# Linear attention and two MLPs: the steps of the second network's weight split set to 1, 4, 7 and 11 of each chunk, its store first in SP's turn, one last store moved to ScalarE's queue

## Chip, cores and metric

The kernel is one program on 1 core of a Trainium2 chip. The metric is the device time of one execution in microseconds (us), the lower the better. Runs of one kernel lie within about 0.2% of each other.

## What is computed

All tensors are float32. Cut to what matters (B = 8 batches, H = 8 heads, S = 576 positions, 64 values per head; 4608 tokens of 512 values; a first network 512 to 2048 to 512, a second 512 to 1024 to 512):

```python
q_s = softmax(q, axis=-1)          # over the 64 values of a head
k_s = softmax(k, axis=2)           # over the 576 positions
kv = einsum('bhsd,bhse->bhde', k_s, v)
x = einsum('bhsd,bhde->bhse', q_s, kv)      # then heads beside each other: 4608 x 512
h = x @ w_in
g = maximum(h, 0) + alpha * minimum(h, 0)
x2 = g @ w_out
h = x2 @ w_in2
sm = softmax(h, axis=-1)
solu = h * sm
ln = (solu - mean(solu)) / sqrt(var(solu) + 1e-6) * g_ln
out = ln @ w_out2
```

## The kernel before, in words

Every large product is made of three matmuls of 128 x 128 by 128 x 512 in float32r: an operand is split into a high half (ScalarE copies it, rounded) and a low half (VectorE or POOL subtracts the high half from the value), and high x high, high x low and low x high are added in PSUM.

The first network's upper product runs in 9 chunks c of 512 tokens, 16 steps f each (`up(c, f)`, lines 1965 to 1967, twelve matmuls). Chunks 0 to 7 hold the first 512 positions of batches 0 to 7, the last one all remainders. A step's result lies in one of four PSUM banks of `ps_y`. ScalarE makes the negative part into `gst` (`negative`, line 993), VectorE adds the rest (`prelu`, line 1421 in the program, called "the negative's sum" below), and SP stores `gst` to `g_scratch` (`store_g`, line 478). `gst` has three buffers: the negative of step f waits until the store of step f - 3 has landed. `up` of step f waits for the sum of step f - 4.

Between the steps of chunks 0 to 6 the attention of the next batch, b = c + 1, is worked on, each engine in an order written out by hand, `for f in range(NF)` with `if f == ...`:

- SP loads K in step 3 (`load_k`), stores qz, the blockwise transposed q, in steps 7 and 8 (`store_qz`, line 500), loads Q of the batch after in step 8 (`load_q`, lines 414 and 419), and loads q back, transposed, as QN in 16 transfers of 64 KB, five each in steps 9 to 11 and the last in step 12 (`load_qz`, line 508). V comes in steps 12 to 15. All of it goes through SP's one queue, in program order; a wait of SP holds whatever follows.
- VectorE makes the q sums in steps 3 and 4 (lines 1387 to 1393), subtracts the maxima of K in step 5 (lines 1345, 1349), transposes q in pairs of blocks in steps 6 and 7 (line 1401), norms kv in step 10 (line 1364), makes kvl in step 11.
- ScalarE makes the exponentials of K in step 7 (`k_exp`, line 940), the two halves of kvh in step 11 (lines 952, 953), copies qR in step 12 (line 959), makes the high halves qTh of q in steps 12 and 13 (`q_high`, line 969).
- POOL makes their low halves qTl (line 812).
- TensorE makes the kv product after step 9 (line 1901), needs the first two of the three K exponentials for it, transposes q's remainder after step 11 (line 1914), multiplies it after step 13 (`xr_product`, line 1950, which needs qR), and makes the attention product in four parts after steps 14 and 15 (`x_product`, lines 1939 to 1941).

Besides, chunks 1 to 6 split the second network's weights, 22 pieces in all, at four steps of each chunk, here called the split. For a piece n, ScalarE makes the high half into `whl` (`ws_high`, lines 1002 and 1004) once the store of piece n - 1 has landed, since `whl` is one buffer; VectorE makes the low half (`ws_low`, lines 1427 and 1430) and for some pieces turns a buffer of weights into a difference (`ws_turn`, lines 1441 and 1450); SP stores both halves, 512 KB, to `ws_scratch` (`store_ws`, line 473) one step later. The raw weights come into `wst` in four loads of 1 MB (`load_ws`, lines 464 and 468), each after the last piece that reads what it overwrites:

```python
WS_AT = (1, 6, 10, 13)
WS_LOADS = {(0, 15): 0, (2, 11): 1, (4, 7): 2, (5, 7): 3}
```

A key (c, f) of the second table is SP's turn in which the load is issued. The pieces 7, 14 and 18 are the first that read the loads 1, 2 and 3. SP's turn of a step ends so:

```python
if f == 15:
    store_xr(b)
if (c, f) in WS_LOADS:
    load_ws(WS_LOADS[c, f])
if ws_piece(c, f - 1) is not None:
    store_ws(ws_piece(c, f - 1))
```

After the chunks come the first network's lower product and the second network, which the change doesn't touch but for the last line: `store_out` (line 687) stores the remainders' output rows, two stores of 64 rows per tile, all from SP. The last tile is made by `out_copy(17, 1)` (line 1191) on ScalarE.

Of the kernel before, what the change touches and what calls it, by code (L numbers as in the profile page):

```python
# [26 lines left out]
def linear_attention_two_mlps(nc, q, k, v, w_in, w_out, alpha, w_in2, w_out2, g_ln, out):  # L27
# [29 lines left out]
    with ExitStack() as ctx:  # L57
# [244 lines left out]
        SUM_AT = {1: 0, 2: 1, 3: 2, 6: 3}  # L302


        WS_AT = (1, 6, 10, 13)
        WS_W2, WS = 14, 14 + NF2
        WS_LOADS = {(0, 15): 0, (2, 11): 1, (4, 7): 2, (5, 7): 3}
        WS_SUMS = (1, 1, 2, 3, 3, 4, 4)

        class Piece:  # L310
# [101 lines left out]
        def _(sp):  # L412
# [119 lines left out]
            for c in range(B - 1):  # L532
                b = c + 1
                for f in range(NF):
                    if c == 0 and f + 4 < NF:
                        load_w(f + 4)
                    if f > 0:
                        store_g(c, f - 1)
                    if c == 0 and 3 <= f <= 7:
# [29 lines left out]
                        store_xr(b)  # L569
                    if (c, f) in WS_LOADS:  # L570
                        load_ws(WS_LOADS[c, f])
                    if ws_piece(c, f - 1) is not None:
                        store_ws(ws_piece(c, f - 1))
                store_g(c, NF - 1)
                if b + 1 < B:
                    load_v_part(b + 1, TT)
# [104 lines left out]
            def store_out(n, t):  # L681
                u, r = pair_at(n)
                sp.wait_ge(o_ok, 2 * n + t + 1)
                if u == PAIRS:
                    for i in range(2):
                        b = 2 * (2 * t + r) + i
                        sp.dma_start(out[b * S + TOK:(b + 1) * S, :], ost[i * REM:(i + 1) * REM, t, :]).then_inc(o_st[t], 16)
                else:
                    rows_out = out.rearrange("(b s) n -> b s n", b=B)[2 * u + t, 0:TOK, :]
                    sp.dma_start(rows_out.rearrange("(p t) n -> p t n", t=TT)[:, r, :], ost[:, t, :]).then_inc(o_st[t], 16)  # L690
# [243 lines left out]
        def _(act):  # L934
# [104 lines left out]
            for c in range(B - 1):  # L1039
                b = c + 1  # L1040
                for f in range(NF):
                    if c == 0 and f + 3 < NF:
                        w_high(f + 3)
                    negative(c, f)
                    if f == (3 if c == 0 else 2):
                        q_exp(b, 0)
                        q_exp(b, 1)
                    if f == (4 if c == 0 else 3):
                        q_exp(b, 2)
                    if f == 7:  # L1050
                        for piece in range(3):
                            k_exp(b, piece)
                    if ws_piece(c, f) is not None:
                        ws_high(ws_piece(c, f))
                    if f == 11:
                        kv_high(b)
                    if f == 12:
                        qr_copy(b)
                    if f == (13 if c == 0 else 12):
                        q_high(b, 0)  # L1060
                        q_high(b, 1)
                    if f == (14 if c == 0 else 13):
                        q_high(b, 2)
                        q_high(b, 3)
                    if f == 14:
                        xr_copy(b)
                        x_high(b, 0)
                        x_high(b, 1)
                    if f == 15:
                        x_high(b, 2)  # L1070
                        x_high(b, 3)
# [216 lines left out]
            out_copy(16, 1)  # L1288
            out_copy(17, 0)
            out_copy(17, 1)  # L1290


        @block.vector
        def _(dve):
# [204 lines left out]
            for c in range(B - 1):  # L1499
                b = c + 1  # L1500
                for f in range(NF):
# [38 lines left out]
                        kv_norm(b)  # L1540
                    if f == 11:
                        kv_low(b)
                    if ws_piece(c, f) is not None:
                        ws_low(ws_piece(c, f))
                        ws_turn(ws_piece(c, f))
                    if c == 0 and f == 13:
                        q_low_second(0)
                        q_low_second(1)
                    if b + 1 < B:
# [4 lines left out]
                            k_rem(b + 1)  # L1554
                        if f == 11:
                            k_blocks(b + 1)
                    if f == 14:
                        x_low(b, 0)
                        x_low(b, 1)
# [586 lines left out]
```

## Time and profile before

| | |
|---|---|
| median of 3 runs | 1207.49 us (1205.42 to 1207.53) |
| the profiled execution's own time | 1208.86 us |
| its span | 1207.1 us |
| TensorE busy | 1187.6 us, 98% |
| VectorE, ScalarE, POOL busy | 74%, 45%, 26% |
| SP's hardware queue | 212.5 MB, 56.4% of 16 engines' span |

Times in the trace count from the span's start. The profiled execution is a fourth one, and the 1.8 us by which its own time exceeds the span lie around the program. PE is TensorE's matmuls, DVE VectorE, ACT ScalarE, SPq the issuing of SP. A matmul's own time of 0.39 us overlaps its neighbours: one starts every 0.227 us at the full clock. "[1.64 <-POOL ...]" is the time that an engine stood idle before an instruction, and what ended it. "To landing" is the time from a DMA's issue to its completion count.

### The profile page before, as it was taken

To read this page: it belongs to the slowest core of one execution; us is meant where nothing else is said; L and a number is where in the kernel's file an instruction comes from. 1 tells how busy PE (TensorE), PEld (TensorE's weight loads), DVE (VectorE), ACT (ScalarE), POOL (GpSimd) and SP (SyncE) were. 2 spreads that over 40 slices of the span, in tenths; PEclk is the share of its full clock that TensorE was granted. 3 is DMA by queue.
4 is the path that set the end of the run, shared out by engine and by line. 5 is a ranking of instruction groups with operands and counts; after the bars stand their busy time and mean duration, and the time that the engine had idled before them with its cause. 6 is when DMAs were issued, how large, how long until landed. Compare 5 with 4: busy or idle time off the path is not lost.

```text
span 1207.1 us, 16162 instructions
## 1 busy us (share of the span) xinstructions
PE 1187.6 (98%) x6013; PEld 982.4 (81%) x6013; DVE 891.2 (74%) x1165; ACT 538.2 (45%) x744; POOL 309.1 (26%) x233
## 2 busy tenths in 40 slices
PE   7999999999999999999999999999999999999998
PEld 6878887887888888888888888898788888888886
DVE  7768777786775475977769777686898787878772
ACT  4534534434354344443444344443556464545452
POOL 5722414132242000000000000036544535353310
PEclk8999999999999999999999999999999999999999
DMA  9998877869874735264270542498346545454444
GB/s 231 255 259 260 244 254 217 271 202 273 270 237 166 266 133 191 96 205 144 83 239 28 189 159 70 142 290 266 122 149 192 176 134 174 136 177 130 145 153 129
DMA packets 211918, 225.07 MB, mean 186 GB/s; under 512 B 63208, under 2 KB 148224, under 8 KB 211712
## 3 DMA queue, kind: packets, MB, share of 16 engines
q1 hardware_dynamic: 206064, 212.50, 56.4%
q0 software_dynamic: 5728, 11.53, 3.3%
q8 instruction: 47, 0.77, 0.3%
q14 instruction: 31, 0.25, 0.1%
q10 hardware_dynamic: 48, 0.01, 0.0%
HBM read 128.51 MB, written 95.48 MB: 186 GB/s over the span
## 4 chain that ended last, share of the span: by engine, by line
PE 83%; DVE 8%; DMA 4%; issue 2%; SPq 2%; ACT 1%; POOL 0%; ACTq 0%; DVEq 0%
PE ps_y L1965 9%; PE ps_y L1966 9%; PE ps_y L1967 9%; PE ps_y L2051 5%; PE ps_y L2053 5%; PE ps_y L2055 5%; PE ps_y L2109 5%; PE ps_y L2111 5%; PE ps_y L2110 5%; PE ps_m L2053 3%; PE ps_m L2055 3%; PE ps_m L2051 3%; PE ps_m L2090 2%; PE ps_m L2094 2%; PE ps_m L2092 2%
## 5 line engine op out<-in xcount | busy, mean ns | idle before, releaser
L1965 PE MATMUL ps_y<-X,W 128*128 128x512 f32 x576 | 227.2, 394 | 0.0
L1967 PE MATMUL ps_y<-X,W 128*128 128x512 f32 x576 | 224.6, 390 | 0.0
L1966 PE MATMUL ps_y<-X,W 128*128 128x512 f32 x576 | 224.6, 390 | 0.0
L1421 DVE SCALAR_TENSOR_TENSOR gst<-gst,nslope,ps_y 128x512 f32<-128x512 f32 x144 | 104.4, 732 | 113.4 <-ACT gst L993 113.0
L993 ACT ACTIVATE gst<-ps_y 128x512 f32<-128x512 f32 x144 | 85.8, 596 | 225.6 <-PE ps_y L1967 166.4
L854 POOL TENSOR_TENSOR x2r<-x2r 128x256 f32<-128x256 f32 x18 | 25.2, 1401 | 406.9 <-DMA x2r<-x_scratch 406.9
L1965 PEld LDWEIGHTS ps_y<-X,W 128*128 128x128 f32 x576 | 108.4, 188 | 23.5
L1967 PEld LDWEIGHTS ps_y<-X,W 128*128 128x128 f32 x576 | 108.3, 188 | 22.9
L1966 PEld LDWEIGHTS ps_y<-X,W 128*128 128x128 f32 x576 | 108.4, 188 | 21.8
L2051 PE MATMUL ps_y<-rh,WOc 128*128 128x512 f32 (+1 forms) x320 | 117.9, 369 | 1.1 <-DVE rl L1583 1.1
L2053 PE MATMUL ps_y<-rl,WOc 128*128 128x512 f32 (+1 forms) x320 | 117.7, 368 | 0.0
L2055 PE MATMUL ps_y<-rh,WOc 128*128 128x512 f32 (+1 forms) x320 | 117.7, 368 | 0.0
L2109 PE MATMUL ps_y<-WO,zh 128*128 128x512 f32 x288 | 112.3, 390 | 1.7 <-DVE zl L1727 1.7
L2111 PE MATMUL ps_y<-WO,zl 128*128 128x512 f32 x288 | 112.1, 389 | 0.0
L2110 PE MATMUL ps_y<-WO,zh 128*128 128x512 f32 x288 | 112.1, 389 | 0.0
L1095 ACT ACTIVATE rh<-RX 128x1024 fp32r<-128x1024 f32 x54 | 57.4, 1062 | 85.8 <-PE ps_y L2055 41.7
L1095 ACT ACTIVATE rh<-RY 128x1024 fp32r<-128x1024 f32 x54 | 57.4, 1062 | 81.6 <-PE ps_y L2055 55.7
L1583 DVE TENSOR_TENSOR rl<-RX,rh 128x1024 fp32r<-128x1024 f32 x54 | 66.2, 1225 | 34.2 <-ACT rh L1095 34.2
L1583 DVE TENSOR_TENSOR rl<-RY,rh 128x1024 fp32r<-128x1024 f32 x54 | 67.4, 1250 | 28.0 <-ACT rh L1095 27.9
L882 POOL TENSOR_TENSOR x2lb<-x2r,x2hb 128x1792 fp32r<-128x1792 f32 x18 | 75.1, 4171 | 41.9 <-ACT x2hb L1130 41.9
L1185 ACT ACTIVATE zh<-zt 128x1024 fp32r<-128x1024 f32 x36 | 38.0, 1056 | 88.4 <-PE ps_y L2111 58.9
L812 POOL TENSOR_TENSOR qTl<-QN,qTh 128x512 fp32r<-128x512 f32 x26 | 33.2, 1298 | 155.3 <-ACT qTh L969 155.3
(189 smaller groups left out, 2534.6 us busy)
## 6 DMA issues: line engine op xcount, KB each, us to landing
g_scratch<-gst SPq DMA_DIRECT2D x144, 256.0 KB, 3.6
RX<-g_scratch SPq DMA_DIRECT2D x36, 512.0 KB, 3.6
z_scratch<-zb SPq DMA_DIRECT2D x36, 512.0 KB, 3.5
zt<-z_scratch SPq DMA_DIRECT2D x144, 128.0 KB, 2.8
ws_scratch<-whl SPq DMA_DIRECT2D x22, 512.0 KB, 4.5
RY<-g_scratch SPq DMA_DIRECT2D x18, 512.0 KB, 4.6
RZ<-g_scratch SPq DMA_DIRECT2D x18, 512.0 KB, 4.7
x2r<-x_scratch SPq DMA_DIRECT2D x18, 512.0 KB, 5.1
```

Source lines behind the costliest of these rows:

```text
L1095: nc.scalar.activation(t.tile(rh), t.raw(src), ACT.Copy).then_inc(bh_ok, 1)
L1421: nc.vector.scalar_tensor_tensor(gst[:, n % 3, :], gst[:, n % 3, :], nslope[:, f:f + 1], ps_y[:, f % 4, :], ALU.mult, ALU.add).then_inc(g_ ...
L1583: nc.vector.tensor_tensor(t.tile(rl), t.raw(src), t.tile(rh).bitcast(F32), ALU.subtract).then_inc(bl_ok, 1)
L1965: nc.tensor.matmul(o, W1[:, f, 0, a, :], x[:, 0, a, :], start=(a == 0), stop=False)
L1966: nc.tensor.matmul(o, W1[:, f, 0, a, :], x[:, 1, a, :], start=False, stop=False)
L1967: mm = nc.tensor.matmul(o, W1[:, f, 1, a, :], x[:, 0, a, :], start=False, stop=(a == KT - 1))
L2051: nc.tensor.matmul(o, WOc[k][:, 0, kt, cols], hi[:, s, :], start=begin, stop=False, skip_group_check=more)
L2053: nc.tensor.matmul(o, WOc[k][:, 0, kt, cols], lo[:, s, :], start=False, stop=False, skip_group_check=more)
L2055: mm = nc.tensor.matmul(o, WOc[k][:, 1, kt, cols], hi[:, s, :], start=False, stop=end, skip_group_check=more)
L2109: nc.tensor.matmul(o, zh[:, t, f * P:(f + 1) * P], WO2[:, f, 0, :], start=(f == 0), stop=False)
L2110: nc.tensor.matmul(o, zh[:, t, f * P:(f + 1) * P], WO2[:, f, 1, :], start=False, stop=False)
L2111: mm = nc.tensor.matmul(o, zl[:, t, f * P:(f + 1) * P], WO2[:, f, 0, :], start=False, stop=(f == NF2 - 1))
```

## The change

The split's four steps move from 1, 6, 10, 13 to 1, 4, 7, 11. The loads 1, 2 and 3 move with the pieces that they wait for: from step 11 of chunk 2 to step 8, from step 7 of chunks 4 and 5 to step 5. SP takes the split's store as the first thing of its turn instead of the last. In ScalarE's step 7 the split's high half now stands ahead of the three K exponentials, and in step 11 behind kvh. VectorE takes the low half behind the K maxima and blocks of its step. At the end one of the four stores of the last two tiles' rows goes out from ScalarE behind its last copy.

```diff
--- before.py
+++ after.py
@@ -302,9 +302,9 @@
         SUM_AT = {1: 0, 2: 1, 3: 2, 6: 3}
 
 
-        WS_AT = (1, 6, 10, 13)
+        WS_AT = (1, 4, 7, 11)
         WS_W2, WS = 14, 14 + NF2
-        WS_LOADS = {(0, 15): 0, (2, 11): 1, (4, 7): 2, (5, 7): 3}
+        WS_LOADS = {(0, 15): 0, (2, 8): 1, (4, 5): 2, (5, 5): 3}
         WS_SUMS = (1, 1, 2, 3, 3, 4, 4)
 
         class Piece:
@@ -534,6 +534,8 @@
                 for f in range(NF):
                     if c == 0 and f + 4 < NF:
                         load_w(f + 4)
+                    if ws_piece(c, f - 1) is not None:
+                        store_ws(ws_piece(c, f - 1))
                     if f > 0:
                         store_g(c, f - 1)
                     if c == 0 and 3 <= f <= 7:
@@ -569,8 +571,6 @@
                         store_xr(b)
                     if (c, f) in WS_LOADS:
                         load_ws(WS_LOADS[c, f])
-                    if ws_piece(c, f - 1) is not None:
-                        store_ws(ws_piece(c, f - 1))
                 store_g(c, NF - 1)
                 if b + 1 < B:
                     load_v_part(b + 1, TT)
@@ -682,7 +682,7 @@
                 u, r = pair_at(n)
                 sp.wait_ge(o_ok, 2 * n + t + 1)
                 if u == PAIRS:
-                    for i in range(2):
+                    for i in range(1 if 2 * n + t == TILES - 1 else 2):
                         b = 2 * (2 * t + r) + i
                         sp.dma_start(out[b * S + TOK:(b + 1) * S, :], ost[i * REM:(i + 1) * REM, t, :]).then_inc(o_st[t], 16)
                 else:
@@ -1047,13 +1047,13 @@
                         q_exp(b, 1)
                     if f == (4 if c == 0 else 3):
                         q_exp(b, 2)
+                    if f == 11:
+                        kv_high(b)
+                    if ws_piece(c, f) is not None:
+                        ws_high(ws_piece(c, f))
                     if f == 7:
                         for piece in range(3):
                             k_exp(b, piece)
-                    if ws_piece(c, f) is not None:
-                        ws_high(ws_piece(c, f))
-                    if f == 11:
-                        kv_high(b)
                     if f == 12:
                         qr_copy(b)
                     if f == (13 if c == 0 else 12):
@@ -1288,6 +1288,8 @@
             out_copy(16, 1)
             out_copy(17, 0)
             out_copy(17, 1)
+            act.wait_ge(o_ok, TILES)
+            act.dma_start(out[B * S - REM:B * S, :], ost[REM:P, 1, :]).then_inc(o_st[1], 16)
 
 
         @block.vector
@@ -1540,9 +1542,6 @@
                         kv_norm(b)
                     if f == 11:
                         kv_low(b)
-                    if ws_piece(c, f) is not None:
-                        ws_low(ws_piece(c, f))
-                        ws_turn(ws_piece(c, f))
                     if c == 0 and f == 13:
                         q_low_second(0)
                         q_low_second(1)
@@ -1554,6 +1553,9 @@
                             k_rem(b + 1)
                         if f == 11:
                             k_blocks(b + 1)
+                    if ws_piece(c, f) is not None:
+                        ws_low(ws_piece(c, f))
+                        ws_turn(ws_piece(c, f))
                     if f == 14:
                         x_low(b, 0)
                         x_low(b, 1)
```

SP's queue in chunk 2, steps 7 to 9, before (ws_scratch is the split's store, g_scratch a step's result, wst the raw weights):

```order
L500 DMA qz_scratch<-qz 128x1024
L473 DMA ws_scratch<-whl 128x2x512
L478 DMA g_scratch<-gst 128x512
L500 DMA qz_scratch<-qz 128x1024
L414 DMA Q<-q_dram 64x8x64
L419 DMA Q<-q_dram 128x4x256 x2
L478 DMA g_scratch<-gst 128x512
L508 DMA QN<-qz_scratch 32x4x128 x5
```

The same now:

```order
L500 DMA qz_scratch<-qz 128x1024
L473 DMA ws_scratch<-whl 128x2x512
L478 DMA g_scratch<-gst 128x512
L500 DMA qz_scratch<-qz 128x1024
L414 DMA Q<-q_dram 64x8x64
L419 DMA Q<-q_dram 128x4x256 x2
L464 DMA wst<-w_in_dram 128x1024 x2
L478 DMA g_scratch<-gst 128x512
L508 DMA QN<-qz_scratch 32x4x128 x5
```

The store stands at the same place but is that of the piece of step 7, no more of step 6; and the two 512 KB loads stand behind Q and ahead of the g store of step 8.

SP's queue in chunk 2, steps 11 and 12, before:

```order
L478 DMA g_scratch<-gst 128x512
L508 DMA QN<-qz_scratch 32x4x128 x5
L464 DMA wst<-w_in_dram 128x1024 x2
L473 DMA ws_scratch<-whl 128x2x512
L478 DMA g_scratch<-gst 128x512
L508 DMA QN<-qz_scratch 32x4x128
```

The same now:

```order
L478 DMA g_scratch<-gst 128x512
L508 DMA QN<-qz_scratch 32x4x128 x5
L473 DMA ws_scratch<-whl 128x2x512
L478 DMA g_scratch<-gst 128x512
L508 DMA QN<-qz_scratch 32x4x128
```

The loads are gone from here; the store ahead of the last QN transfer is that of the piece of step 11 instead of step 10.

ScalarE in chunk 4, steps 4 to 11, before (gst are the negatives, whl the split's high half, KK the K exponentials, kvh the two halves of kv):

```order
L993 ACTIVATE gst<-ps_y 128x512 x3
L1002 ACTIVATE whl<-wst 128x512
L993 ACTIVATE gst<-ps_y 128x512
L940 ACTIVATE KK<-KK 64x512
L940 ACTIVATE KK<-KK 128x1024 x2
L993 ACTIVATE gst<-ps_y 128x512 x3
L1004 ACTIVATE whl<-wst,acols 128x512
L993 ACTIVATE gst<-ps_y 128x512
L952 ACTIVATE kvh<-kvf 64x4x64
L953 ACTIVATE kvh<-kvf 64x4x64
```

The same now:

```order
L993 ACTIVATE gst<-ps_y 128x512
L1002 ACTIVATE whl<-wst 128x512
L993 ACTIVATE gst<-ps_y 128x512 x3
L1004 ACTIVATE whl<-wst,acols 128x512
L940 ACTIVATE KK<-KK 64x512
L940 ACTIVATE KK<-KK 128x1024 x2
L993 ACTIVATE gst<-ps_y 128x512 x4
L952 ACTIVATE kvh<-kvf 64x4x64
L953 ACTIVATE kvh<-kvf 64x4x64
L1004 ACTIVATE whl<-wst,acols 128x512
```

The first piece that reads load 2 has moved from step 10 to step 7, ahead of the K exponentials, and a further one stands behind kvh in step 11.

## Rows read from the trace of the kernel before

**Rows 1.** Windows, chunks 1, 2, 4, 5: length, busy, PEclk, DMA share, GB/s
```profile
85.14:136.59 51.45, 51.45 (x305) 41.89 (x304) 40.25 (x58) 21.98 (x38) 14.94 (x10) 1.00 0.87 266
136.59:192.09 55.50, 53.57 (x305) 42.87 (x304) 38.60 (x57) 21.87 (x38) 15.16 (x10) 0.97 0.79 244
...
243.55:295.87 52.32, 51.55 (x305) 41.89 (x304) 39.73 (x56) 22.04 (x39) 15.19 (x10) 1.00 0.82 249
295.87:347.57 51.70, 51.54 (x305) 41.89 (x304) 37.58 (x55) 22.35 (x38) 15.19 (x10) 1.00 0.83 257
```

**Rows 2.** Timeline of TensorE, chunks 2 and 4: start, us, operation, idle
```profile
176.22 0.68 PE L1950 MATMUL ps_m<-qR,kvf 64*64 64x64 f32 x16
...
185.57 0.50 PE L1939 MATMUL ps_m<-qTh,kvh 128*128 128x512 f32 x1 [1.64 <-POOL qTl L812]
...
188.27 0.63 PE L1965 MATMUL ps_y<-X,W 128*128 128x512 f32 x1
...
267.92 3.58 PE L1901 MATMUL ps_m<-V,KK 128*64 128x65 f32 x80
...
277.95 0.46 PE L1914 MATMUL ps_m<-ident,QN 64*128 64x64 f32 x4 [0.78 <-DVE kvf L1364]
```

**Rows 3.** Timeline of ScalarE, chunk 2, steps 11 to 13
```profile
170.25 0.60 ACT L993 ACTIVATE gst<-ps_y 128x512 f32<-128x512 f32 x1 [1.60 <-PE ps_y L1967]
170.75 0.40 ACT L952 ACTIVATE kvh<-kvf 64x256 fp32r<-64x256 f32 x1
...
174.10 0.38 ACT L959 ACTIVATE qR<-ps_m 128x256 f32<-128x256 f32 x1
...
181.37 0.63 ACT L1002 ACTIVATE whl<-wst 128x512 fp32r<-128x512 f32 x1 [4.44 <-DMA ws_scratch<-whl]
183.54 1.15 ACT L969 ACTIVATE qTh<-QN 128x512 fp32r<-128x512 f32 x2 [1.55 <-DMA QN<-qz_scratch]
```

**Rows 4.** Chain that ended last, chunks 2 and 4: start, us, what
```profile
175.59 7.93 DMA QN<-qz_scratch
...
266.58 9.10 DMA g_scratch<-gst
```

**Rows 5.** Timeline of SP's queue, chunk 2
```profile
158.31 0.37 SPq L473 DMA_DIRECT2D ws_scratch<-whl  x1
...
173.66 0.91 SPq L464 DMA_DIRECT2D wst<-w_in_dram  x2
```

**Rows 6.** Windows within chunk 2, columns as in rows 1
```profile
161.00:170.00 9.00, 9.00 (x105) 7.36 (x104) 4.68 (x8) 1.72 (x3) 0.00 (x0) 1.00 0.98 302
170.00:176.00 6.00, 6.00 (x29) 4.75 (x28) 5.80 (x9) 3.34 (x7) 0.78 (x1) 1.00 0.79 219
```

**Rows 7.** Timeline of VectorE, chunks 2 and 4
```profile
157.64 0.64 DVE L1427 TENSOR_TENSOR whl<-wst,whl 128x512 fp32r<-128x512 f32 x1
...
159.47 1.28 DVE L1401 STREAM_TRANSPOSE qz<-QN 128x512 f32<-128x512 f32 x2
...
258.00 0.65 DVE L1421 SCALAR_TENSOR_TENSOR gst<-gst,nslope,ps_y 128x512 f32<-128x512 f32 x1
```

**Rows 8.** DMA issues, 163 to 164 and 265 to 265.7: us to landing
```profile
g_scratch<-gst SPq DMA_DIRECT2D x1, 256.0 KB, 6.4
...
wst<-w_out_dram SPq DMA_DIRECT2D x1, 1024.0 KB, 6.8
```

**Rows 9.** DMAs issued in 1202 to 1208
```profile
out_dram<-ost SPq DMA_DIRECT2D x4, 128.0 KB, 2.4
```

**Rows 10.** Timeline of ScalarE, chunks 4 and 5
```profile
261.85 0.60 ACT L993 ACTIVATE gst<-ps_y 128x512 f32<-128x512 f32 x1 [4.10 <-DMA g_scratch<-gst]
...
263.34 2.52 ACT L940 ACTIVATE KK<-KK 64x512 f32<-64x512 f32 x3
...
312.90 0.60 ACT L993 ACTIVATE gst<-ps_y 128x512 f32<-128x512 f32 x1 [2.83 <-DMA g_scratch<-gst]
```

**Rows 11.** Timeline of SP's queue at the end
```profile
1202.48 2.38 SPq L687 DMA_DIRECT2D out_dram<-ost  x4
```

## The prediction

> **What bounds the kernel now.** I began with the windows by chunk, because the change touches only the first network's chunks 1 to 6 and the very end. A chunk that nothing disturbs takes 51.45 us and TensorE is busy in all of it [rows 1]: there the matmuls set the time, and no work saved on another engine is worth anything. Chunk 2 takes 55.50, chunk 4 52.32 and chunk 5 51.70. Above 51.45 that is 4.05, 0.87 and 0.25, together 5.17 us. This is all that a better order of steps could give back there; chunks 1, 3 and 6 can only lose.
>
> Next, where the 5.17 us arise. In chunk 2 TensorE stands 1.64 us before the product of step 15, which waits for qTl, and soon after, single matmuls take 0.63 us where 0.39 was usual: the granted clock fell to half [rows 2]. Behind the wait stands ScalarE: the high half of the weight split of step 13 idles 4.44 us for the split's last store, then qTh idles 1.55 us for a transfer of QN, and only then can POOL make qTl [rows 3]. That transfer, the sixteenth of its kind, was issued at 175.59 and took 7.93 us to land [rows 4], since SP had put two 512 KB loads at 173.66 ahead of it [rows 5]. In chunk 4 it is a g store that took 9.10 us behind the 1 MB load: the negative of step 10 waited for it, and through it the kv norm and the transpose at 277.95, before which TensorE stood 0.78 us [rows 2, 4]. Chunk 5 repeats it, milder. So SP's queue and the 16 DMA engines are the true second resource: they are busy 0.98 of the time from 161 to 170 [rows 6].
>
> **Part 1, what goes away.** No split stands between the negative of step 13 and qTh of chunk 2 any more, and the load leaves step 11: the 1.64 us wait and the half clock lose their cause, 4.05 us. The 1 MB loads of chunks 4 and 5 leave step 7, so that the g store that step 10 needs isn't behind them: 0.87 and 0.25 us. No bytes are removed and no instruction is cheaper; all is moved.
>
> **Part 2, the new waits in chunk 2.** SP issues in order, so a store that comes first in its turn holds everything behind it until VectorE has made its low half. In step 8 this store now belongs to the piece of step 7, whose low half comes after the second pair of transposes. The pair ends at 159.47 + 1.28 = 160.75 as before (the piece's low half and the turn behind it moved from ahead of it to step 4), the low half 0.64 later [rows 7], so the store goes out at about 161.4 and not 158.31 [rows 5]: 3.1 us later, and with it the g store of step 7, qz, the Q loads and the g store of step 8. Before, the latter was issued in the stretch 163 to 164 and took 6.4 us [rows 8], so it landed at 170.1. The engines were at 0.98 [rows 6], so a shift is hardly absorbed; I take 2.1 of the 3.1 (some slack lay ahead of 159). Then the new load lies before it: a 1 MB load took 6.8 us to land [rows 8], of which some 2 us are the way of any transfer here (the last stores of the kernel, 128 KB each, took 2.4 [rows 9]), so it occupies 2.4 to 4.4; I take 3.4. The g store of step 8 lands at 170.1 + 2.1 + 3.4 = 175.6. The negative of step 11 needs its buffer: 175.6 and not 170.25 [rows 3]. Behind it on ScalarE come two halves of kvh (the first 0.40), now also the split's high half (0.63), the negative of step 12 (0.60) and the copy to qR (0.38 [rows 3]); as each starts some 0.1 before the last one ends, 2.8 us. TensorE wants qR at 176.22 [rows 2], so the point is a landing at 173.4, and at 175.6 it stands 2.2 us (bounds 0, if the load is absorbed, and 3.9). Behind it the last QN transfer follows the store of the piece of step 11, which waits for a low half that is itself late: about 0.5 us at the product of step 15 (0 to 1). Whether the clock halves after a wait of 2.2 us is open: it did after 1.64 us and didn't after the 0.78 us of chunk 4 [rows 2]. At eight matmuls by about 0.2 us it is 1.6, and I count half, 0.8. Chunk 2: 2.2 + 0.5 + 0.8 = 3.5 us in place of 4.05.
>
> **Part 3, the new waits in chunks 4 and 5.** The load at step 5 can only follow the low half of step 4's piece: VectorE reaches the negative's sum of step 5 at 258.00 [rows 7], the low half now goes in ahead of it, so the store is issued at 258.7, the g store of step 4 behind it, the load at 259.5. The queue is then behind the K loads: the g store of step 3 landed at 261.85 [rows 10]. After it store and g store need about 2 us, the load 2.4 to 4.4: it lands at 266.3 to 268.3, mean 267.3. ScalarE now makes the high half of that piece in step 7 ahead of the three K exponentials (2.52 us [rows 10]), where before it made them from 263.34 with no wait. TensorE's kv product starts at 267.92 [rows 2] and needs the first two, 2.1 us after the load with the split's 0.6. So 267.3 + 2.1 = 269.4, a stand of 1.4 us (0 to 2.4). In chunk 5 the g store of step 3 landed 17.0 us into the chunk against 18.3 in chunk 4 [rows 1, 10], 1.3 earlier, and the kv product starts at the same place: 0.2 us (0 to 1.1). Chunk 1 has the same shift of step 8 without a load: 0.1 us (0 to 0.5).
>
> Here a rule speaks otherwise. The row has 6.8 us for 1 MB behind a half full queue. The Trainium skill, DMA: Bandwidth & Descriptors, section Anatomy of one DMA, gives a fixed 2.0 us plus the bytes at 436 GB/s, an estimate of 4.4 us for 1 MB, while its section Bandwidth lists 6.15 us measured; the trace agrees with the second. By the first, both the loads' new places would be harmless in chunks 4 and 5.
>
> **Part 4, the last rows.** SP issues four stores of 128 KB one after the other from 1202.48, 2.38 us in all, each landing 2.4 us later [rows 9, 11]. One of them now goes from ScalarE, whose last copy they wait for. The last landing moves up by one issue, 2.38 / 4 = 0.6 us (0 if both queues share the issuing hardware, which no row shows).
>
> **Sum.** Before 5.17. After: 3.5 + 1.4 + 0.2 + 0.1 = 5.2. The chunks stay as they are, the end gives 0.6. The sum is made against the profiled execution, 1208.86 us (span 1207.1 and 1.8 around it), 1.37 above the median of 1207.49: 1208.3 on its scale, 1206.9 on the median's. About 0.2%, 2.4 us, is what can be told from no change: faster means below 1205.1, slower above 1209.9.
>
> **The rivals.**
> 1. The queue drains. The load at step 8 and the later stores find gaps, since the bytes are spread better than in a row at 173.66. At 2.4 us for the load and no delay of the negative of step 11, all chunks run at 51.45: 5.17 + 0.6 less, 1201.7; with a rest of 1.2 + 0.5 us in chunk 2 it is 1203.4. For it: from 170 to 176, with the qz loads being issued, the engines were at 0.79 [rows 6]. Against: 0.98 in just the stretch that the load enters [rows 6]. Chance 0.30.
> 2. The queue doesn't drain, and the kernel is slower. One mechanism: the negative of step 11 of chunk 2 waits for the g store behind Q and the load. It decides at 173.4; at 177.3 TensorE stands 3.9 us, the clock halves (1.6) and 0.5 follows, 6.0 in place of 4.05; with the loads' upper bound the K exponentials cost 2.4 and 1.1 too and chunk 1 0.1. Then 9.6 - 5.17 - 0.6 = +3.8: 1211.3. For it: in chunk 4 a g store with a load and a split's store just ahead took 9.10 us [rows 4]. Chance 0.20.
> 3. The change doesn't do what it says: the split's bytes still lie ahead of the last QN transfer, which lands no earlier than 183.5, and only the 0.6 us of the end are left: 1206.9. Chance 0.05, within the no-change band.
>
> **How the numbers follow.** The forecast, waits that move from one place to another, has 0.45, with a range of its own of 1204.5 to 1209.5. Faster is rival 1 and a small part of the forecast, 0.33. Slower is rival 2 and a small part, 0.22. The rest is 0.45. The range leaves out the lowest tenth (chunks wholly clean on a lucky chip) and the highest: 1202.0 to 1210.5. I name 1206.9.
>
> **What would show it.** In the windows by chunk, chunk 2 at about 55, chunk 4 near 52.8, chunk 5 near 51.7, chunk 1 within 0.3 of 51.45. In chunk 2 no idle of qTh behind the split; instead an idle of several us before the negative of step 11 with a g store as its releaser, and a TensorE gap before the product into qR's buffer. In chunks 4 and 5 the high half of step 7 ends an idle behind the 1 MB load, and the kv product starts over 1 us late in chunk 4. At the end three stores from SP and one from ScalarE. The prediction is wrong if the negative of step 11 starts before 173.4 in chunk 2's own time (36.8 us into it), or if the half clock appears in chunk 4.

## The result, and the profile after

| | before | after |
|---|---|---|
| median (range, runs) | 1207.34 us (1205.42 to 1207.53, 4) | 1221.11 us (1216.93 to 1222.97, 4) |
| the profiled execution, its span | 1208.86, 1207.1 us | 1216.93, 1215.1 us |

The change makes the kernel slower, by a ratio of 1.0113 with an interval of 1.0084 to 1.0142: some 14 us where I had forecast none. The profiled execution of the changed kernel is the fastest of its four and that of the kernel before lies 1.5 us above its median, so the traces show only 8.0 us of it. The windows of the changed kernel, chunks 1 to 6 in order, with the columns of [rows 1]:

```profile
84.84:138.30 53.46, 52.09 (x305) 41.74 (x304) 40.59 (x58) 21.41 (x39) 15.46 (x10) 1.00 0.84 254
138.30:195.46 57.16, 54.18 (x305) 43.93 (x304) 40.76 (x57) 21.75 (x38) 15.91 (x10) 0.94 0.77 239
195.46:247.44 51.98, 51.85 (x305) 41.84 (x304) 38.95 (x57) 21.70 (x38) 15.51 (x10) 1.00 0.78 237
247.44:300.50 53.06, 51.62 (x305) 41.81 (x304) 40.23 (x56) 22.07 (x38) 15.94 (x10) 1.00 0.81 251
300.50:355.71 55.21, 51.97 (x305) 41.73 (x304) 38.12 (x55) 21.99 (x38) 15.97 (x10) 1.00 0.80 245
355.71:407.16 51.45, 51.45 (x305) 41.88 (x304) 30.35 (x48) 21.24 (x36) 15.51 (x10) 1.00 0.48 160
```

Nearly all of it is in these chunks. Against [rows 1], chunk 1 is 2.01 us longer, chunk 2 1.66, chunk 4 0.74 and chunk 5 3.51; chunk 3, which ran at 51.46 before, is 0.52 longer. That is 8.4; chunk 1 starts 0.30 earlier than before and all that follows chunk 6 is 0.13 shorter, its gain of 0.5 at the very end included, so the spans differ by 8.0. TensorE's busy time exceeds 51.45 by 2.73 us in chunk 2 and by at most 0.64 in the others, where most of the loss is standing. Where it waits, in the timeline of TensorE, twice in chunk 1, then in chunks 2, 4 and 5:

```profile
110.01 2.20 PE L1903 MATMUL ps_m<-V,KK 128*64 128x65 f32 x47 [0.73 <-ACT KK L940]
...
133.32 0.50 PE L1941 MATMUL ps_m<-qTh,kvh 128*128 128x512 f32 x1 [0.35 <-POOL qTl L812]
...
180.97 1.12 PE L1952 MATMUL ps_m<-qR,kvf 64*64 64x64 f32 x16 [2.98 <-issue]
182.02 0.79 PE L1967 MATMUL ps_y<-X,W 128*128 128x512 f32 x1
182.62 0.63 PE L1968 MATMUL ps_y<-X,W 128*128 128x512 f32 x1
...
273.32 1.83 PE L1903 MATMUL ps_m<-V,KK 128*64 128x65 f32 x40 [1.44 <-ACT KK L940]
...
327.91 3.58 PE L1903 MATMUL ps_m<-V,KK 128*64 128x65 f32 x80 [2.96 <-ACT KK L940]
```

The 1.64 us wait for qTl of [rows 2] is gone from chunk 2. In its place stand 2.98 us ahead of the product that needs qR (line 1952 is line 1950 of before), with the half clock behind it, and a wait for the K exponentials in chunks 1, 4 and 5. The K exponentials are less than half of chunk 1's loss: its kv product (line 1903) starts 0.80 us late, and the remaining 1.2 us come later in the chunk, where TensorE stands 0.35 and 0.28 us for qTl at step 15; for the rest the trace names no wait. A window from 180 to 187 has a granted clock of 0.51, the 1.2 GHz level. It costs at most what TensorE's busy time in chunk 2 exceeds 51.45 by, 2.73 us (in chunk 1 that excess is 0.64 at the full clock), and 2.98 + 2.73 is the 5.71 by which the chunk is longer than 51.45.

The timeline of ScalarE, chunks 1, 2 and 5, tells who was late:

```profile
105.48 0.60 ACT L993 ACTIVATE gst<-ps_y 128x512 f32<-128x512 f32 x1 [4.44 <-DMA g_scratch<-gst]
107.38 0.60 ACT L993 ACTIVATE gst<-ps_y 128x512 f32<-128x512 f32 x1 [1.30 <-DMA g_scratch<-gst]
107.87 0.62 ACT L1002 ACTIVATE whl<-wst 128x512 fp32r<-128x512 f32 x1
108.39 2.51 ACT L940 ACTIVATE KK<-KK 64x512 f32<-64x512 f32 x3
...
178.14 0.60 ACT L993 ACTIVATE gst<-ps_y 128x512 f32<-128x512 f32 x1 [8.30 <-DMA g_scratch<-gst]
...
180.50 0.37 ACT L959 ACTIVATE qR<-ps_m 128x256 f32<-128x256 f32 x1
...
187.88 1.15 ACT L969 ACTIVATE qTh<-QN 128x512 fp32r<-128x512 f32 x2 [5.49 <-DMA QN<-qz_scratch]
...
325.67 0.72 ACT L1004 ACTIVATE whl<-wst,acols 128x512 fp32r<-128x512 f32 x1 [5.08 <-DMA wst<-w_out_dram]
326.30 2.51 ACT L940 ACTIVATE KK<-KK 64x512 f32<-64x512 f32 x3
```

The negative of step 11 in chunk 2 starts at 178.14, 39.84 us into the chunk, where it was 33.66 before [rows 1, 3]. In chunk 5 the split's high half waits for the 1 MB load and the K exponentials stand behind it. In chunk 1, where no load is moved, the negatives of steps 6 and 7 each wait for a g store and the exponentials start at 108.39. The wait at step 6 was there before; the second one, 1.30 us, is new. The DMAs that end these waits, by time of issue (169.5 to 170, then 316.4 to 316.9), columns as in [rows 8]:

```profile
g_scratch<-gst SPq DMA_DIRECT2D x1, 256.0 KB, 8.5
...
wst<-w_out_dram SPq DMA_DIRECT2D x1, 1024.0 KB, 9.2
```

The g store is that of step 8. Before, it was issued 27.09 us into chunk 2:

```profile
163.68 0.51 SPq L478 DMA_DIRECT2D g_scratch<-gst  x1
```

Now it is 31.27 us into the chunk, 4.2 later. The split's store goes out 25.13 us into it and not 21.72 [rows 5], and the load stands ahead of the g store:

```profile
163.43 0.37 SPq L473 DMA_DIRECT2D ws_scratch<-whl  x1
...
168.55 0.98 SPq L464 DMA_DIRECT2D wst<-w_in_dram  x2
169.57 0.46 SPq L478 DMA_DIRECT2D g_scratch<-gst  x1
```

And why the last transfer of QN is late in chunk 2, in the timeline of SP's queue:

```profile
177.10 2.35 SPq L508 DMA_DIRECT2D QN<-qz_scratch  x5
183.32 0.38 SPq L473 DMA_DIRECT2D ws_scratch<-whl  x1
183.74 0.47 SPq L478 DMA_DIRECT2D g_scratch<-gst  x1
184.26 0.84 SPq L508 DMA_DIRECT2D QN<-qz_scratch  x1
```

and in the timeline of VectorE:

```profile
178.77 0.75 DVE L1423 SCALAR_TENSOR_TENSOR gst<-gst,nslope,ps_y 128x512 f32<-128x512 f32 x1 [4.75 <-ACT gst L993]
...
180.40 0.71 DVE L1317 STREAM_TRANSPOSE kmt<-kmax 128x512 f32<-128x512 f32 x1
181.14 0.69 DVE L1321 TENSOR_REDUCE kx<-kmt 128x16 f32<-128x512 f32 x1
181.75 1.54 DVE L1429 TENSOR_TENSOR whl<-wst,whl 128x512 fp32r<-128x512 f32 x1
```

SP issues nothing from 179.45 to 183.32. It holds its turn 12 for the split's store, which needs the low half; that now stands behind kvl and the K maxima and blocks, and these follow the late step 11. So a late g store makes the low half late, the low half makes SP late, and SP makes QN late. In chunk 2 this costs TensorE nothing, since it is late enough itself; the waits for qTl at step 15 of chunk 1 are of this kind.

### The profile page after: what moved, and what is told of

Same layout as the page of the kernel before. It is cut to its first block, busy times and chain, and to the rows that moved or that the text cites. A ratio compares the mean times of both kernels' runs of the same rounds, so it can differ in the third digit from the quotient of the medians.

```text
span 1215.1 us, 16162 instructions
## 1 busy us (share of the span) xinstructions
PE 1190.2 (98%) x6013; PEld 983.0 (81%) x6013; DVE 894.8 (74%) x1165; ACT 536.4 (44%) x744; POOL 311.4 (26%) x233
## 4 chain that ended last, share of the span: by engine, by line
PE 82%; DMA 6%; DVE 6%; issue 2%; SPq 2%; ACT 1%; POOL 1%; ACTq 0%; DVEq 0%
PE ps_y L1967 8%; PE ps_y L1969 8%; PE ps_y L1968 8%; PE ps_y L2053 5%; PE ps_y L2057 5%; PE ps_y L2055 5%; PE ps_y L2111 5%; PE ps_y L2113 5%; PE ps_y L2112 5%; PE ps_m L2053 3%; PE ps_m L2057 3%; PE ps_m L2055 3%; DMA g_scratch<-gst 2%; PE ps_m L2092 2%; PE ps_m L2096 2%; PE ps_m L2094 2%
```

## The experiments

Four runs of the changed kernel are few where the ratio is to be split up, so it is measured once more. All ratios are to the kernel before, run beside it on the same chip; kernels of different chips are compared by their ratios. Chunk lengths are windows of one profiled execution each. A chunk can differ by 1 to 3 us between executions, with the same code (chunk 2 is 55.50 in [rows 1] and 52.69 in the kernel that has only the tail changed, chunk 5 51.70 and 53.41), so the table's ratio has the last word.

| kernel | median (runs) | ratio [95%] | chunks 1 to 5 |
|---|---|---|---|
| after, again | 1218.05 (4) | 1.0094 [1.0077, 1.0110] | 54.44 55.35 51.45 53.04 56.61 |
| tail only | 1207.26 (10) | 0.9997 [0.9988, 1.0006] | 51.45 52.69 51.45 52.26 53.41 |
| exponentials first | 1215.06 (4) | 1.0056 [1.0040, 1.0073] | 54.60 54.92 51.72 53.91 55.61 |
| store last | 1213.33 (8) | 1.0051 [1.0032, 1.0070] | 51.45 52.42 51.45 55.79 54.37 |
| before, store first | 1212.81 (10) | 1.0044 [1.0027, 1.0060] | 51.56 55.26 51.45 54.29 53.29 |
| both orders back | 1204.80 (10) | 0.9982 [0.9969, 0.9994] | 51.45 52.84 51.45 51.46 51.45 |
| small loads | 1209.07 (10) | 1.0019 [1.0004, 1.0035] | 53.08 53.06 51.68 51.48 52.38 |
| loads at chunk ends | 1203.24 (10) | 0.9970 [0.9958, 0.9981] | all 51.45 or 51.46 |
| only turn 12 last | 1210.38 (10) | 1.0012 [0.9995, 1.0029] | 51.75 53.61 51.46 51.45 51.45 |
| turns 2, 5, 8 last | 1208.38 (10) | 0.9997 [0.9981, 1.0013] | 51.74 54.48 51.46 53.44 51.46 |
| loads at ends, again | 1203.29 (7) | 0.9960 [0.9945, 0.9974] | all 51.45 or 51.46 |

**The changed kernel again**, unedited.

> The changed kernel itself, unedited, beside the others. Theory A (late landings behind the moved 1 MB loads: the negative of step 11 in chunk 2, the K exponentials in chunks 4 and 5): the profile shows the same three TensorE gaps, of 3.1, 1.6 and 3.1 us give or take 1.5, and the median is 1217 to 1223. Theory B (SP's queue held by the store that stands first in its turn) expects the same total but also losses in the chunks without a load, 1 and 3, of 2.0 and 0.5 us.

It is slower by 0.94%, 11 us, within the interval of the first comparison. Chunk 1 loses 3.0 us here and chunk 3 nothing, so of theory B's two signs one comes and the other doesn't come again. Chunk 2 stands 2.3 us for qR with no half clock behind it. In chunk 5 the same wait for the K exponentials is 2.06 us here and the half clock follows it. TensorE's timeline:

```profile
326.48 5.28 PE L1903 MATMUL ps_m<-V,KK 128*64 128x65 f32 x80 [2.06 <-ACT KK L940]
331.69 0.80 PE L1967 MATMUL ps_y<-X,W 128*128 128x512 f32 x1
332.28 0.63 PE L1968 MATMUL ps_y<-X,W 128*128 128x512 f32 x1
```

The same 80 matmuls took 3.58 us in the first profile. The waits are of the same kinds in both executions; the half clock moves about.

**The tail alone**, in the kernel before:

```diff
-                    for i in range(2):
+                    for i in range(1 if 2 * n + t == TILES - 1 else 2):
...
+            act.wait_ge(o_ok, TILES)
+            act.dma_start(out[B * S - REM:B * S, :], ost[REM:P, 1, :]).then_inc(o_st[1], 16)
```

> The kernel before with only the last store moved to ScalarE's queue. Both theories: chunks as before, last landing 0.6 us earlier relative to the last copy, 1206.7 (0.0 to 0.8 us below the kernel before).

0.9997: no difference that can be told, and none is needed. In the traces the span ends 5.2 us after the start of the last copy before and 4.7 after, in this kernel and in the changed one: 0.5 us. The loss isn't here.

**The K exponentials ahead of the split's high half**, in the changed kernel:

```diff
+                    if f == 7:
+                        for piece in range(3):
+                            k_exp(b, piece)
                     if f == 11:
                         kv_high(b)
                     if ws_piece(c, f) is not None:
                         ws_high(ws_piece(c, f))
-                    if f == 7:
-                        for piece in range(3):
-                            k_exp(b, piece)
```

> The changed kernel with the K exponentials of step 7 ahead of the split's high half again. Theory A: the kv products of chunks 4 and 5 start 24.4 us into their chunks again, which gives back 1.6 + 3.1 us, and most of the 0.8 us of chunk 1; chunk 2 keeps its loss; in all 4 to 6 us below the changed kernel. Theory B: the low half and the store get no earlier, so SP is held as long; 0 to 2 us below the changed kernel.

It gives back 0.38% of the 0.94%. The kv product starts 24.37 us into chunks 4 and 5, where an undisturbed one does, so their wait is gone. But these chunks are no shorter: now TensorE stands for qR (0.9 us in chunk 4) and for qTl at the products of step 15 (0.6 and 0.3 us there), and in chunk 5 the clock falls behind that. TensorE's timeline, chunk 5:

```profile
348.24 0.50 PE L1941 MATMUL ps_m<-qTh,kvh 128*128 128x512 f32 x1 [1.35 <-POOL qTl L812]
...
350.30 0.63 PE L1967 MATMUL ps_y<-X,W 128*128 128x512 f32 x1
```

The wait that the change had removed from chunk 2 is back, in chunk 5. A second delay lay hidden behind the first: the last QN transfer that SP holds. The six chunks sum to 322.2 us here and to 322.3 in either profile of the changed kernel, so these traces don't show where the 0.38% lies.

**The store last again in SP's turn**, in the changed kernel:

```diff
-                    if ws_piece(c, f - 1) is not None:
-                        store_ws(ws_piece(c, f - 1))
                     if f > 0:
                         store_g(c, f - 1)
...
                     if (c, f) in WS_LOADS:
                         load_ws(WS_LOADS[c, f])
+                    if ws_piece(c, f - 1) is not None:
+                        store_ws(ws_piece(c, f - 1))
```

> The changed kernel with SP's store of the split last in its turn again. Theory A: loads still precede the g store of step 8 in chunk 2 and are at most 1 us earlier in chunks 4 and 5; at most 2 us below the changed kernel. Theory B: the g stores of steps 4, 7 and 11 and the last QN transfer no longer wait for VectorE's low half; chunks 1 and 3 return to 51.45, and the kernel is 4 us or more below the changed one.

It gives back 0.43%. Chunks 1 and 3 are clean at once, and chunk 2 drops to 52.42. Chunks 4 and 5 keep their wait for the exponentials, 2.9 us in each, with the half clock behind the one in chunk 4: together the whole of their loss. In chunk 4 the high half ahead of them no longer waits for the load but for the split's last store, which stands behind the load and takes 9.4 us to land. Of all of TensorE's waits, this one is the largest sum, as in the changed kernel (engine and line, for whom; us in all, times, longest):

```profile
PE ps_m L1903 <- ACT KK L940: 5.7, 2, 2.9
```

How the store did it in chunk 1 is seen on ScalarE, where the steps' negatives 6 and 7 run together, with no second wait:

```profile
104.23 1.20 ACT L993 ACTIVATE gst<-ps_y 128x512 f32<-128x512 f32 x2 [5.47 <-DMA g_scratch<-gst]
106.07 0.63 ACT L1002 ACTIVATE whl<-wst 128x512 fp32r<-128x512 f32 x1 [0.64 <-DMA ws_scratch<-whl]
106.61 2.51 ACT L940 ACTIVATE KK<-KK 64x512 f32<-64x512 f32 x3
```

Store first in turn 5 makes the g store of step 4 wait for VectorE's low half of the same step, and the negative of step 7 needs that g store's buffer: the 1.30 us of the changed kernel. There SP issues nothing from 98.15 to 100.59:

```profile
97.30 0.85 SPq L478 DMA_DIRECT2D g_scratch<-gst  x1
100.59 0.37 SPq L473 DMA_DIRECT2D ws_scratch<-whl  x1
101.01 2.06 SPq L478 DMA_DIRECT2D g_scratch<-gst  x2
```

**The store first, alone**, in the kernel before (the two hunks of the change in SP's turn, nothing else).

> The kernel before with nothing changed but the split's store first in SP's turn; steps 1, 6, 10, 13 and the loads as before. If the store's place in SP's turn does harm by itself, chunks 1, 3 and 6 grow: the store of step 10 holds the g store and the transfers of step 11 until VectorE's low half, and the kernel is 1 to 4 us slower. If it does harm only with the steps 4, 7, 11, where the low half comes behind other work of VectorE, it is within 1 us of the kernel before.

1.0044: 5 us lost by the order in SP's turn alone, with the old steps and the old order on ScalarE. But not where I expected it: chunks 1, 3 and 6 stay at 51.45 to 51.56, and the trace has the loss in chunks 4 and 5, where TensorE now stands 1.2 and 1.3 us for the kv norm and in chunk 4 also 1.5 us for qR. Engine and line, for whom; us in all, times, longest:

```profile
PE ps_m L1914 <- DVE kvf L1364: 2.5, 2, 1.3
```

So the store's place does harm in both kernels, but the loss of chunk 1 comes only with the new steps.

**Both orders back, new steps and new loads kept**: the edits of exponentials first and of store last on the changed kernel together.

> The changed kernel with both orders undone: SP's store last in its turn, the K exponentials ahead of the split's high half. What is left of the change is the steps 1, 4, 7, 11, the three moved loads and ScalarE's last store. Expected if the two orders carry the loss: chunks 1 and 3 at 51.45, kv products at 24.4 us, chunk 2 about 52.4, chunks 4 and 5 below 53; 1204 to 1208. If the moved loads carry it through other waits: chunks 4 and 5 above 54, 1210 to 1214.

0.9982, with an interval that ends at 0.9994: what is left of the change, the steps, the loads' new turns and the tail, is a small gain. Chunks 4 and 5 are clean, and chunk 2 has 52.84 with the 1 MB in step 8. TensorE's waits in this kernel have no qTl and no exponentials; in chunks 1 to 6 only the product that needs qR stands, 1.3 us in chunk 2 (the other of the two times is ahead of these chunks):

```profile
PE ps_m L1952 <- issue: 1.9, 2, 1.3
```

The negative of step 11 starts 38.18 us into chunk 2 and not 39.84.

**Small loads**, in the changed kernel. It leaves out most of the raw weights of these loads, so the pieces from 7 on split old data; only its time counts:

```diff
+                        if n == 0:
...
+                            sp.dma_start(wst[:, 2 * half, 0:64], w_in2[row:row + P, 0:64]).then_inc(ws_in[n], 16)
...
-                    sp.dma_start(wst[:, :, :], w_out2[row:row + 4 * P, :].rearrange("(a p) n -> p a n", p=P)
-                                 ).then_inc(ws_in[n], 16)
+                    sp.dma_start(wst[:, 0, 0:64], w_out2[row:row + P, 0:64]).then_inc(ws_in[n], 16)
```

> The changed kernel with loads 1, 2 and 3 cut from 1 MB to 64 or 32 KB each: the rest of the raw weights is left out, so the pieces 7 to 21 split old data. If the bytes of the loads make the losses of chunks 2, 4 and 5: the kv products at 24.4 us, the negative of step 11 in chunk 2 near 36, chunks 2, 4 and 5 like chunk 3, 5 to 8 us below the changed kernel. If the held SP queue makes them: chunk 1 stays near 54, and the kernel is at most 3 us below the changed one.

1.0019: the bytes of three loads, 3 MB, are worth 0.75% of the changed kernel's 0.94%, 9 us, more than either branch of the expectation had. The kv product starts on time in chunks 4 and 5 even with the exponentials behind the high half, so that order is dear only with a load to wait for. Chunk 1 keeps 53.08 (53.46 and 54.44 with the loads): it never had a load, only the store. In chunk 2 the negative of step 11 starts 36.78 us into the chunk, and TensorE doesn't stand for qR, only 0.6 and 0.3 us for qTl.

**Loads at the ends of the chunks**, on the kernel before with the new tail. Step 13 of chunks 2 and 4 makes no piece, so that the loads can go out where SP's queue has less to do:

```diff
-        WS_LOADS = {(0, 15): 0, (2, 11): 1, (4, 7): 2, (5, 7): 3}
+        WS_LOADS = {(0, 15): 0, (2, 14): 1, (4, 14): 2, (5, 15): 3}
+        WS_SLOTS = [(c, f) for c in range(1, 7) for f in WS_AT if (c, f) not in ((2, 13), (4, 13))]
...
-            if c > 0 and f in WS_AT and 4 * (c - 1) + WS_AT.index(f) < WS:
-                return Piece(4 * (c - 1) + WS_AT.index(f))
+            if (c, f) in WS_SLOTS:
+                return Piece(WS_SLOTS.index((c, f)))
```

> The kernel before with the pieces on the steps 1, 6, 10, 13, but step 13 of chunks 2 and 4 left free, so that the loads 1, 2 and 3 go out in step 14, 14 and 15 of chunks 2, 4 and 5, behind the last transfer of q, like load 0; and ScalarE's last store. If the 1 MB loads in the middle of the chunks are what costs, all chunks run at 51.45 and it is 4 to 6 us below the kernel before, 1202 to 1204. If contention merely moves, one of chunks 3, 5, 6 grows and it is within 1 us of it.

All six chunks run at the 51.45 us of [rows 1]. The windows of chunks 2 and 5:

```profile
135.84:187.30 51.46, 51.46 (x305) 41.89 (x304) 37.31 (x55) 21.70 (x38) 15.20 (x10) 1.00 0.82 252
...
290.20:341.66 51.46, 51.46 (x305) 41.89 (x304) 37.49 (x55) 22.37 (x39) 15.20 (x10) 1.00 0.80 249
```

DMA is as busy as before in chunks 2 and 5 (0.79 and 0.83 in [rows 1]); no byte is saved, and TensorE never stands in these chunks. The ratio is 0.9970 and, measured again, 0.9960: this version beats both kernels. The edit does two things, though: it moves the loads, and it takes the piece out of step 13 of chunks 2 and 4, whose high half stood ahead of qTh in [rows 3]. How much each of them gives no run separates.

**Which turn of the store**: both kernels have the exponentials first; one moves only turn 12's store to the turn's end, the other only those of turns 2, 5 and 8.

```diff
-                    if ws_piece(c, f - 1) is not None:
+                    if (f != 12) and ws_piece(c, f - 1) is not None:
...
+                    if not (f != 12) and ws_piece(c, f - 1) is not None:
+                        store_ws(ws_piece(c, f - 1))
```

(in the second kernel with f == 12 in place of f != 12)

> The changed kernel with the K exponentials first again, and of SP's stores only that of step 11's piece put back to the end of its turn (turn 12); those of turns 2, 5 and 8 stay first. If SP is held mainly in turn 12, between the fifteenth and the last QN transfer, the waits for qTl before the attention product vanish and it comes to 1206 to 1209, of the 10 us between 1215 and 1205 more than half. If it is held mainly in turns 5 and 8, ahead of the g stores, it is at most 3 us below 1215.

> The counterpart: the store of step 11's piece stays first in turn 12, those of turns 2, 5 and 8 go to the end. If turn 12 carries the loss, it stays at 1211 to 1215 with TensorE waiting for qTl; if turns 5 and 8 do, it comes to 1205 to 1208. With both parts real and independent, the two kernels' gains against 1215.1 add up to 10.3 us.

From the 1.0056 with all four stores first, turn 12 alone gives back 0.44% and turns 2, 5 and 8 0.59%, while all four give back 0.74% (both orders back). So neither place is the one cause; each gives more than half (1210.4 us for the first lies a little above what I expected). The traces tell the two apart by the wait. With turn 12's store last TensorE never stands for qTl, but 2.1 us for qR in chunk 2; with the other three last it stands for qTl in chunks 2 and 4 (0.7 and 0.8 us at the longest) and 1.5 us for qR in chunk 2. Chunk 1 drops from 54.60 to 51.75 and 51.74, so its loss seems to need both. That the two gains add up to more than 0.74% would fit a loop in which a late step 11 delays the store of turn 12 and that store delays QN, but the intervals, 0.17% to either side of each ratio, don't rule out that they just add. One of the ten runs of the first kernel took 5789 us and no other came near it; the ratio leaves it out, and without it the median is 1209.78.

**The loads at the ends once more**, beside these.

> The kernel with the loads at the chunks' ends once more, in more rounds: 1203.2 give or take 0.7, all chunks 1 to 6 at 51.45, ratio to the kernel before 0.997 with an interval clear of 0.999.

0.9960, 4.7 us by medians, with 4.0 the first time.

## Why the prediction was wrong, point by point

- **The step that failed.** Against clean chunks of 51.45 the prediction had waits of 3.5 (chunk 2), 1.4 (4), 0.2 (5) and 0.1 us (1), together 5.2. The first profile has 5.7, 1.6, 3.8, 2.0 and 0.5 in chunk 3, together 13.6. Two terms make 5.5 of the 8.4 us that are missing: the 0.2 of chunk 5, a load's landing taken from another transfer, and the 0.1 of chunk 1, where the hold of the store that now comes first was not followed. The medians differ by 13.8 us, not by the 8.0 of the two traces; no profile shows where the rest lies.
- **The bound.** 51.45 us per clean chunk was right, and 5.17 us to be won came near. The version with the loads at the chunk ends has every chunk clean and wins 4.0 and 4.7 us by medians, tail included.
- **Part 1.** In the first profile the wait for qTl in chunk 2 and the waits for the kv norm in chunks 4 and 5 are gone, as said. In the second the wait for qTl is there again, 0.69 and 0.29 us in chunk 2.
- **Part 2, chunk 2: right mechanism, each size a little short.** The g store of step 8 was to land 39.0 us into the chunk and did at 39.8; TensorE stood 2.98 and not 2.2. I took 2.1 of the store's 3.1 us of delay as passed on; with small loads the negative still starts 3.1 us later than before (36.78 against 33.66), so none was absorbed. The load came to about 3.1 more, where I had 3.4; but with the load in place and the store last again it is 38.18, so the two overlap. The clock was halved for 6.8 us (0.51 in the mean over 7.0) and not for the 3.4 of eight matmuls, and cost up to 2.73 where I had 0.8: I counted half of a price read from one earlier case. In the second profile the clock didn't fall in this chunk. The 0.5 at step 15 didn't come: qTh waited 5.49 us for the last QN transfer, but TensorE was by then late enough itself, and the trace has no further wait of it in this chunk. 57.16 against 54.95: 2.2 us too little. Two bounds there have no working: the load's lower one, 2.4 us, comes from no row (1 MB at the 302 GB/s of [rows 6] takes 3.5), and 177.3 isn't 170.1 + 3.1 + 4.4, which is 177.6.
- **Part 3, chunk 4: right.** 1.44 us against 1.4, with the high half and its load as the releaser. The load went out 16.03 us into the chunk and took 7.6, so it landed at 23.6; I had 23.75 (267.3).
- **Part 3, chunk 5: the largest error in the trace.** I had 0.2, from the g store of step 3 landing 1.3 us earlier than in chunk 4. The load went out 15.96 us into the chunk, to 0.01 us where I had put it, and then took 9.2 us. I had it land at 23.75 - 1.3 = 22.45, which allows 6.5. A landing 1.3 us earlier of another transfer, in a kernel whose queue the change fills differently, was no measure of this queue. In the prediction's terms it is the load's landing that was mis-sized. The wait was 2.96, and 2.06 with the half clock behind it in the other execution: chunk lengths of 55.21 and 56.61 against 51.65.
- **Chunk 1: the step that failed in kind.** "Chunk 1 has the same shift of step 8 without a load: 0.1 us (0 to 0.5)". It lost 2.0 in one profile and 3.0 in the other. I had followed the store's hold in turn 8, and in turn 12 for chunk 2 alone; never in turn 5, where it delays the g store that the negative of step 7 needs, with the K exponentials behind it, and never in turn 12 of this chunk, where it delays the last QN transfer and with it qTl. Small loads leave 1.6 us of chunk 1's loss, so most of it isn't a matter of the loads. The store last again makes it clean, and so do the old steps with the store first (51.56): it takes the new steps and the store first together.
- **The sum as a form.** I priced the two new orders each by itself, against an otherwise unchanged queue. Taken back alone they give 0.38% and 0.43%, together 1.12% (1.0094 to 0.9982). That is 0.31% more than the sum, which the intervals (0.12 to 0.19% to either side of each of the four ratios) only just allow to be noise. It is what one expects where the longest of several waits decides and behind it the next stands ready, as chunk 5 showed with the exponentials first.
- **Part 4.** 0.6 forecast, 0.5 in the trace. The Trainium skill, DMA: Bandwidth & Descriptors, section Issuing engines are not separate DMA queues, says that issuing from several engines saves only the issue time. The last store lands 2.7 us after its issue from ScalarE against 2.5 from SP, so the trace agrees: what is saved is one issue, not a transfer.
- **The rivals.** Rival 2 had the right sign, with 3.8 us where the medians have 10.5 and 13.8: it took the bounds of my terms, and the terms that failed (chunk 1, chunk 5) lay outside theirs. My signs of being wrong didn't show: the negative of step 11 started after 36.8 us in both profiles of the changed kernel (39.84 and 39.13), and the half clock wasn't in chunk 4. They tested chunk 2 and the clock, not the terms that failed. Rival 1, the queue that drains, comes near only when both orders are taken back: 1204.80, with a rest of 1.4 us in chunk 2 where its second form (1203.4) had 1.7. Even then the negative of step 11 is 4.5 us later than before, so the queue doesn't drain as it said.
- **The page's rule.** The fit of the Trainium skill, DMA: Bandwidth & Descriptors, section Anatomy of one DMA, a fixed 2.0 us plus the bytes at 436 GB/s, gives an estimate of 4.4 us for 1 MB. The page measured it on DMAs issued from GpSimd, and these go out from SP. The trace differs, and decides: 6.8 us in [rows 8], 7.6 in chunk 4 and 9.2 in chunk 5 of the changed kernel. I was right to prefer the row, and wrong to use it as a constant.

## What to carry to other kernels

In an in-order queue, ask of a store moved to the front of a turn not how long it takes but whom its wait stops: follow it in every turn in which it occurs, and through each small ring of buffers (here three `gst`) to the engine that needs the next one. Price a transfer in a loaded queue with a range as wide as the trace shows for its like, and price moved waits as a chain, not as a sum, since taking one away can show the next. Where bytes can't be saved, move them to the stretch in which nobody waits for the queue.

## What the hardware did that I hadn't expected

The last stores of the changed kernel, 1210.5 to 1216:

```profile
out_dram<-ost SPq DMA_DIRECT2D x3, 128.0 KB, 2.5
out_dram<-ost ACTq DMA_DIRECT2D x1, 128.0 KB, 2.7
```

Both queues issue at the same time with next to no cost to each other: the three of SP take 1.75 us, 0.58 each, where the four took 2.38 [rows 11], 0.60 each. SP's issuing itself isn't of constant length: the qz store at 164.36 in chunk 2 held SP for 1.98 us, where the one at 161.01 took 0.32:

```profile
161.01 0.32 SPq L500 DMA_DIRECT2D qz_scratch<-qz  x1
...
164.36 1.98 SPq L500 DMA_DIRECT2D qz_scratch<-qz  x1
```

And the half clock doesn't follow from the length of a stand alone. It came behind 1.64 us (before, chunk 2), 2.98 (after, chunk 2), 2.06 (after again, chunk 5) and 1.35 with 0.28 (exponentials first, chunk 5), but not behind 1.44 (after, chunk 4) nor behind 2.96 in chunk 5 of the first profile, at the very place where 2.06 brought it in the other. With the store last it came behind 2.86 us in chunk 4 and not behind 2.85 in chunk 5, at the same product in the same execution. What decides no run here shows. It may be part of why the changed kernel's first median lies 4 us above its fastest run: the mean clock of that run is 0.994, and 0.990, 0.993 and 0.990 in the others.
